# Attention on one Trainium2 core: V stationary, the work behind exp one tile later, and the output scaled by GpSimd

## The chip, the cores and the metric

The kernel runs on one NeuronCore of one Trainium2 chip. The metric is the device time of one execution in microseconds (us), the median of several runs. All durations of single instructions come from one profiled execution of the kernel before.

## What is computed

An attention over buckets, then two mixture-of-experts layers on its output. The change touches the attention alone, cut here to what matters:

```python
batch, n_heads, seq, head_dim = (2, 8, 768, 64)     # q, k, v float32; proj is 64 x 6
q_bits = (np.einsum('bhsd,dk->bhsk', q, proj) > 0)  # k_bits the same from k
mask = q_bucket[:, :, :, None] == k_bucket[:, :, None, :]
scores = np.where(mask, scale * np.matmul(q, k.transpose(0, 1, 3, 2)), -1000000000.0)
attn = np.exp(scores - np.max(scores, axis=-1, keepdims=True))
attn = attn / (np.sum(attn, axis=-1, keepdims=True) + 1e-09)
out = np.matmul(attn, v)
```

Behind it come a layer of 8 experts with two per token and one of 8 experts with one per token, over 1536 tokens of 512 values.

## The kernel before

There are H = 16 pairs of batch and head, treated one after another ("head" below). A head has 768 rows of q, taken as QT = 6 tiles of 128 rows; n counts tiles over all heads, j within a head. Head 0 and head 15 are written out, the 14 between run in a loop of two heads a round (over_heads). Each engine has its own program, and the order within it is the order written; engines meet by semaphores.

For a tile, TensorE computes 128 x 768 scores into one of two PSUM banks (scores, L1059 and L1060: two matmuls for each half of 384 columns, in fp32r, where each value is held as a high and a low part). The bits of the bucket are further rows of the same product, so that scores of other buckets come out very negative. VectorE takes the row maximum and makes the scale and bias from it (stats, L722, L725, L728). ScalarE computes exp with the row sum (expo, L561) into one of two buffers "probs" (in the tile work). TensorE transposes the six 128 x 128 blocks of it into one PSUM tile (turn, L1071); ScalarE copies the first half to SBUF (evac, L569), and VectorE the second half in even tiles (L735), ScalarE in odd ones. Then TensorE multiplies by V (weigh, L1083): for each of six blocks, the transposed P block of 128 x 128 is the stationary operand and V, 128 x 64 in plain fp32, moves; an fp32 product is two instructions. After six tiles VectorE scales the whole head's output by the inverse row sums into x_sb (head_out, L749; the inverses at L739 and L741).

Between these, the next head is prepared in six units, one per tile (prep_unit, PREP): the units for k and q (two halves each) are three transposes (L1039), a copy of the high part by ScalarE (L554) and a subtraction for the low part by VectorE (L702, L706); each of q and k is loaded twice, side by side, so that the transposed rows fill both halves of the partitions. The last two units compute the sign bits of the projections by four matmuls (L1044 to L1048), and VectorE turns them into rows of the operands (L710, L713). GpSimd copies the high part of q once more (q_copy, L453).

On TensorE the order of a tile is: scores(n), prep unit j of the next head, weigh(n - 2), turn(n - 1). On VectorE: stats, inverse sums, prep unit, head_out, evac. On ScalarE: copy of the prep unit, exp, evac. SP's queue issues the loads of q and k of the head after next (L328), the load of V (L331), and once in two heads the clears: 1 MB and 0.5 MB to xs (L352) and 1 MB to ys (L348), from a tile of zeros. After the last head, the routing of the first layer starts once x_sb is written; ScalarE and GpSimd then split the first expert's weights (L618, L463).

## Time and profile before

| | us |
|---|---|
| median of 3 runs | 1034.82 (1034.65 to 1037.06) |
| the profiled execution | 1035.75 |
| its span, first to last instruction | 1033.9 |
| PE busy in the span | 936.5 |
| VectorE busy | 587.9 |
| GpSimd busy | 410.1 |
| ScalarE busy | 340.3 |
| attention, first scores to the last write of x_sb | 16.95 to 347.63 |

The profiled execution is 1.85 us longer than its span. Busy time is the union of an engine's instructions. PE is TensorE's matmuls, PEld its weight loads, which overlap them; DVE is VectorE, ACT ScalarE, POOL GpSimd, SP the engine that issues most DMAs. A matmul's end in the trace is modelled, so the distance from one start to the next is the better measure of what it costs in a stream. L and a number is a line of the kernel before.

### The profile page before, as it was taken

The numbers are of one execution on the slowest core, as the hardware profiler recorded it, in microseconds if no ns is written. First come the engines' busy times: TensorE is split into PE (matmuls) and PEld (weight loads), VectorE is DVE, ScalarE is ACT, GpSimd is POOL, SyncE is SP. The second block draws the span as 40 slices with busy tenths as digits, with TensorE's granted clock in tenths as the row PEclk, the third lists the DMA queues.
The fourth block names the chain that finished last, engine by engine and source line by source line (L and its number), as shares of the span: only waits on it lengthen the run. The fifth ranks groups of instructions, "written<-read, shape, count | busy, mean of one in ns | idle before, by whom it ended". The sixth has DMA issues, their size and how long they took to land. (4 is left out here: it accounts for less than half of the span.)

```text
span 1033.9 us, 19204 instructions
## 1 busy us (share of the span) xinstructions
PE 936.5 (91%) x5502; PEld 793.0 (77%) x5503; DVE 587.9 (57%) x1136; ACT 340.3 (33%) x548; POOL 410.1 (40%) x251
## 2 busy tenths in 40 slices
PE   6999999999999938999999999999854999999980
PEld 4889988988898726888888888888643788888860
DVE  5777777777777474544445544454367454444432
ACT  2655555565555410422121111120212134342000
POOL 1000000000000547966152433331955889896004
PEclk9999999999999967999999999999976999999995
DMA  8351543435514525655252534332765677774107
GB/s 264 95 156 38 147 138 70 139 89 124 142 38 171 203 98 207 238 191 189 75 181 84 170 102 141 122 131 87 231 210 189 216 239 254 234 252 147 47 31 243
DMA packets 116173, 158.31 MB, mean 153 GB/s; under 512 B 57904, under 2 KB 59952, under 8 KB 116144
## 3 DMA queue, kind: packets, MB, share of 16 engines
q1 hardware_dynamic: 83280, 70.37, 22.3%
q10 hardware_dynamic: 26624, 67.12, 19.9%
q0 software_dynamic: 6240, 20.45, 6.1%
q8 instruction: 16, 0.26, 0.1%
q14 instruction: 13, 0.11, 0.0%
HBM read 104.43 MB, written 53.48 MB: 153 GB/s over the span
## 5 line engine op out<-in xcount | busy, mean ns | idle before, releaser
L463 POOL TENSOR_TENSOR wring<-stage,wring 128x1024 f32 (+1 forms) x128 | 302.3, 2395 | 197.1 <-ACT wring L618 197.0
L618 ACT ACTIVATE wring<-stage 128x1024 f32 (+1 forms) x128 | 135.4, 1061 | 429.7 <-POOL wring L463 213.8
L1203 PE MATMUL bank<-wring,xT_hl 128*128 x352 | 142.7, 405 | 5.2 <-DVE xT_hl L936 5.2
L1083 PE MATMUL bank<-raw,work 128*128 128x64 f32 x1152 | 143.6, 275 | 3.2 <-ACT work L569 3.2
L1083 PEld LDWEIGHTS bank<-raw,work 128*128 128x128 f32 x1152 | 135.9, 191 | 12.9 <-issue 10.9
L1220 PE MATMUL bank<-wring,hT_hl 128*128 x352 | 141.6, 402 | 3.2 <-DVE hT_hl L955 3.2
L453 POOL TENSOR_TENSOR wring<-wring,ones 64x384 fp32r<-64x384 f32 x32 | 26.2, 819 | 287.3 <-ACT wring L554 287.3
L1205 PE MATMUL bank<-wring,xT_hl 128*128 x352 | 138.8, 394 | 0.0
L1204 PE MATMUL bank<-wring,xT_hl 128*128 x352 | 137.9, 392 | 0.0
L1222 PE MATMUL bank<-wring,hT_hl 128*128 x352 | 137.8, 391 | 0.0
L1221 PE MATMUL bank<-wring,hT_hl 128*128 x352 | 137.1, 390 | 0.0
L962 DVE COPY work<-bank 128x512 f32<-128x512 f32 x44 | 30.5, 694 | 178.2 <-PE bank L1222 168.5
L561 ACT ACTIVATE work<-bank,stat 128x768 f32<-128x768 f32 x96 | 95.2, 991 | 101.8 <-DVE stat L728 101.8
L722 DVE TENSOR_REDUCE stat<-bank 128x1 f32<-128x768 f32 x96 | 91.8, 956 | 59.7 <-PE bank L1060 58.5
L943 DVE TENSOR_SCALAR work<-bank 128x512 f32<-128x512 f32 x88 | 60.9, 692 | 108.2 <-PE bank L1205 108.2
L1203 PEld LDWEIGHTS bank<-wring,xT_hl 128*128 128x128 f32 x352 | 66.8, 190 | 18.6 <-issue 6.2
L1071 PE MATMUL bank<-ident,work 128*128 128x128 f32 x576 | 79.9, 275 | 0.6 <-ACT work L569 0.6
L1220 PEld LDWEIGHTS bank<-wring,hT_hl 128*128 128x128 f32 x352 | 66.1, 188 | 16.1 <-issue 3.7
L1205 PEld LDWEIGHTS bank<-wring,xT_hl 128*128 128x128 f32 x352 | 66.6, 189 | 14.8
L1222 PEld LDWEIGHTS bank<-wring,hT_hl 128*128 128x128 f32 x352 | 66.1, 188 | 14.7
L1204 PEld LDWEIGHTS bank<-wring,xT_hl 128*128 128x128 f32 x352 | 67.0, 190 | 13.0
L1221 PEld LDWEIGHTS bank<-wring,hT_hl 128*128 128x128 f32 x352 | 66.3, 188 | 12.7
(171 smaller groups left out, 1290.6 us busy)
## 6 DMA issues: line engine op xcount, KB each, us to landing
stage<-in_moe_w_dram ACTq DMA_DIRECT2D x128, 512.0 KB, 4.0
ys<-work SPq DMA_DIRECT2D x44, 256.0 KB, 3.4
work<-xs SPq DMA_DIRECT2D x40, 256.0 KB, 3.5
xs<-stage SPq DMA_DIRECT2D x7, 1024.0 KB, 4.5
ys<-stage SPq DMA_DIRECT2D x7, 1024.0 KB, 8.2
raw<-in_k_dram SPq DMA_DIRECT2D x32, 192.0 KB, 3.6
raw<-in_q_dram SPq DMA_DIRECT2D x32, 192.0 KB, 3.8
xs<-stage SPq DMA_DIRECT2D x7, 512.0 KB, 5.2
```

Of the source, the lines that this page charges most:

```text
L463: nc.gpsimd.tensor_tensor(wring[:, bass.ds(at + DC * F, GW)], stage[:, j % STAGES, :], wring[:, bass.ds(at, GW)].bitcast(F32), ALU.subtrac ...
L561: nc.scalar.activation(probs[par].rearrange("p (b c) -> p b c", b=2), s_ps[par][:, :, 0:HALF], ACT.Exp, bias=stat[:, par, 2:3], scale=stat ...
L618: nc.scalar.activation(wring[:, bass.ds(parity * SLOT + high_at(j), GW)], stage[:, j % STAGES, :], ACT.Copy).then_inc(w_high, 1)
L722: vec.tensor_reduce(stat[:, par, 0:1], s_ps[par][:, :, 0:HALF], AX.XY, ALU.max).then_inc(s_max, 1)
L1071: ins = nc.tensor.transpose(pt_ps[:, half, i * P:(i + 1) * P], probs[par][:, c:c + P], ident[:])
L1083: ins = mm(o_ps[:, j * D:(j + 1) * D], probsT[j % 2][:, i * P:(i + 1) * P], vraw[:, hp, i], start=i == 0, stop=i == QT - 1)
L1203: mm(o, xT_hl[:, 0, c, :], wh, start=c == 0, stop=False)
L1204: mm(o, xT_hl[:, 0, c, :], wl, start=False, stop=False)
L1205: ins = mm(o, xT_hl[:, 1, c, :], wh, start=False, stop=c == DC - 1)
L1220: mm(y_ps[:], hT_hl[:, 0, c, :], wh, start=c == 0, stop=False)
L1221: mm(y_ps[:], hT_hl[:, 0, c, :], wl, start=False, stop=False)
L1222: ins = mm(y_ps[:], hT_hl[:, 1, c, :], wh, start=False, stop=c == FC - 1)
```

## The change

V is split by GpSimd into a high and a low part side by side (v_hl, 128 columns) and becomes the stationary operand; three tiles' transposed P, also split into high and low (pT_top by ScalarE, pT_rest by VectorE), moves, 384 columns at a time. The result is the transposed output of three tiles, its two halves of 64 partitions to be added. ScalarE copies it (o_copy), a product with the matrix "fold" transposes it back and adds the halves (turn_back), ScalarE copies that out of PSUM (o_evac), and GpSimd scales it into x_sb (head_out). turn, the evacuations and all behind them run for tile n - 2 where they ran for n - 1. q and k are loaded once, side by side, and transposed together in two units; the high and low parts are put in their places by seven DMAs from SBUF to SBUF per head (put_split, put_bits), for which the first scores of a head wait. The sign bits take three matmuls per half and one VectorE instruction. The maximum is taken negated, and its product with the scale is a tensor_tensor. The parts of the diff that matter are these, added lines alone, less indented; what they take the place of stands in the functions printed above (semaphore names and the constants of the start are left out):

```diff
+qk_raw = raw[:, 0:2].rearrange("p a t d -> p (a t d)").rearrange("p (t x) -> p t x", x=2 * D)
...
+qk_top = ring_part(11)
+qk_rest = ring_part(12)
+late = wring[:, SLOT:2 * SLOT]
+TRIO = 3 * P
+pT_top = [late[:, i * QT * TRIO:(i + 1) * QT * TRIO].rearrange("p (c n) -> p c n", n=TRIO) for i in (0, 1)]
+pT_rest = [late[:, i * QT * TRIO:(i + 1) * QT * TRIO].rearrange("p (c n) -> p c n", n=TRIO) for i in (2, 3)]
+v_hl = [late[:, (16 + i) * S:(17 + i) * S].rearrange("p (c x) -> p c x", x=2 * D) for i in range(2)]
...
+o_flat = [work[:, 2 * S + i * TRIO:2 * S + (i + 1) * TRIO] for i in range(2)]
+fold = work[:, 3 * S:3 * S + D]
+o_raw = [work[:, 3 * S + D + i * KH * D:3 * S + D + (i + 1) * KH * D].rearrange("p (t d) -> p t d", d=D)
+         for i in range(2)]
...
+o_ps = banks[3][:, 0, 0:TRIO]
+misc_ps = banks[3][:, 1, :]
...
+U = 4
+PUTS = 7
+S_O0 = 2
...
+        for at, t in ((0, q), (D, k)):
+            sp.dma_start(qk_raw[:, :, at:at + D], head_rows(t, h)).then_inc(qk_ld, 16)
+    def put(to, at, n, t, row):
+        sp.dma_start(to[at:at + n, :].bitcast(F32), t[row:row + n, :].bitcast(F32)).then_inc(qk_put, 16)
+    def put_split(h, par):
+        sp.wait_ge(prep_ev, h * U + 2)
+        put(q_hl[par], 0, D, qk_top, 0)
+        put(k_hh[par], 0, D, qk_top, D)
+        put(q_hl[par], D, D, qk_rest, 0)
+        put(k_hh[par], D, D, qk_top, D)
+        put(q_hb[par], 0, D, qk_top, 0)
+        put(k_lb[par], 0, D, qk_rest, D)
+    def put_bits(h, par):
+        sp.wait_ge(prep_ev, h * U + 4)
+        put(q_hb[par], D, 2 * BITS, k_lb[par], QB)
...
+    put_split(0, 0)
+    put_bits(0, 0)
+    def next_head(h, par):
+        put_split(h + 1, 1 - par)
+        load_qk(h + 2)
+        put_bits(h + 1, 1 - par)
+        sp.wait_ge(v_rdy, h * 2 + 2)
+        load_v(h + 2, par)
+            next_head(i * 2 + par, par)
+    put_split(H - 1, 1)
+    put_bits(H - 1, 1)
...
+    def split_v(h, par, part):
+        c = slice(part % 2 * KH, (part % 2 + 1) * KH)
+        vr = vraw[:, par, c]
+        if part < 2:
+            if part == 0:
+                pool.wait_ge(v_ld[par], (h // 2) * 16 + 16)
+                if not (isinstance(h, int) and h < 2):
+                    pool.wait_ge(s_pv, h * 2 - 2)
+            one = ones[:, 0:KH * D].rearrange("p (c d) -> p c d", d=D) if KH * D <= P else \
+                ones[:, 0:1].unsqueeze(1).broadcast_to([P, KH, D])
+            nc.gpsimd.tensor_tensor(v_hl[par][:, c, 0:D], vr, one, ALU.mult).then_inc(v_top, 1)
+        else:
+            pool.wait_ge(v_top, h * 2 + (part - 1))
+            nc.gpsimd.tensor_tensor(v_hl[par][:, c, D:2 * D], vr, v_hl[par][:, c, 0:D].bitcast(F32),
+                                    ALU.subtract).then_inc(v_rdy, 1)
+    def head_out(h, hp, half):
+        pool.wait_ge(o_out, h * 2 + (half + S_O0 + 1))
+        pool.wait_ge(s_rinv, h * 2 + 2)
+        xs = x_sb[:].rearrange("p b t h d -> p (b t) (h d)")
+        to = xs[:, bass.ds(h // HB * QT + half * KH, KH), bass.ds(h % HB * D, D)]
+        nc.gpsimd.tensor_tensor(to, o_raw[half],
+                                rinv[:, hp, half * KH:(half + 1) * KH].unsqueeze(2).broadcast_to([P, KH, D]),
+                                ALU.mult).then_inc(s_o, 1)
+    def head(h, hp):
+        for j in range(4):
+            split_v(h, hp, j)
+        if not first(h):
+            for half in range(2):
+                head_out(h - 1, 1 - hp, half)
+    over_heads(pool, head)
+    for half in range(2):
+        head_out(H - 1, 1, half)
...
+    def top_part(h, u):
+        act.wait_ge(prep_mm, h * U + (u + 1))
+        nc.scalar.activation(qk_top[:, cols(u)], prep_bank(h, u)[:, 0:HALF], ACT.Copy).then_inc(prep_top, 1)
...
+    def pT_high(n, hh, j):
+        for half in range(2):
+            act.wait_ge(pt_mm, n * 2 + (half + 1))
+            if half == 0 and not (isinstance(hh, int) and hh < 2):
+                act.wait_ge(s_pv, hh - 1)
+            at = j % KH * P
+            nc.scalar.activation(pT_top[j // KH][:, half * KH:(half + 1) * KH, at:at + P],
+                                 pt_ps[:, half, 0:HALF].rearrange("p (c n) -> p c n", n=P),
+                                 ACT.Copy).then_inc(pt_top, 1)
+    def o_copy(hh, par):
+        act.wait_ge(s_pv, hh + 1)
+        nc.scalar.activation(o_flat[par], o_ps, ACT.Copy).then_inc(o_cp, 1)
+    def o_evac(hh, half):
+        act.wait_ge(o_back, hh + 1)
+        act.wait_ge(s_o, hh + (S_O0 - 1))
+        nc.scalar.activation(o_raw[half], misc_ps[:, 0:KH * D].rearrange("p (t d) -> p t d", d=D),
+                             ACT.Copy).then_inc(o_out, 1)
+    for u in range(2):
+        top_part(0, u)
+            if j >= 2:
+                pT_high(n - 2, h * 2 + (j - 2) // KH, j - 2)
+            elif not first(h):
+                pT_high(n - 2, h * 2 - 1, QT - 2 + j)
+            if j in (1, 4) and not first(h):
+                o_copy(h * 2 - (2 if j == 1 else 1), 0 if j == 1 else 1)
+            if not last(h) and j < 2:
+                top_part(h + 1, j)
+            if not first(h) and j >= U:
+                o_evac(h * 2 - 2 + (j - U), j - U)
...
+    link(vec.tensor_tensor(fold, ident[:, 0:D], ident[:, D:P], ALU.add))
...
+        half = u % 2
+        if u < 2:
+            dve.wait_ge(prep_top, h * 2 + (u + 1))
+            ins = vec.tensor_tensor(qk_rest[:, c], bank[:, 0:HALF], qk_top[:, c].bitcast(F32), ALU.subtract)
+            b = slice(D, PW)
+            ins = vec.tensor_scalar(k_lb[par][b, c], bank[b, 0:HALF], bit_rule[b, 2:3], bit_rule[b, 3:4],
+                                    ALU.is_gt, ALU.mult)
...
+        vec.tensor_reduce(stat[:, par, 0:1], s_ps[par][:, :, 0:HALF], AX.XY, ALU.max,
+                          negate=True).then_inc(s_max, 1)
+        dve.wait_ge(s_max, n + 1)
+        vec.tensor_scalar(stat[:, par, 1:2], stat[:, par, 0:1], BIG / 2, SCALE, ALU.is_lt,
+                          ALU.mult).then_inc(s_scale, 1)
+        dve.wait_ge(s_scale, n + 1)
+        vec.tensor_tensor(stat[:, par, 2:3], stat[:, par, 0:1], stat[:, par, 1:2],
+                          ALU.mult).then_inc(s_stat, 1)
+    def pT_low(n, j):
+        dve.wait_ge(pt_top, n * 2 + 2)
+        at = j % KH * P
+        vec.tensor_tensor(pT_rest[j // KH][:, :, at:at + P].rearrange("p (b c) n -> p b c n", b=2),
+                          pt_ps[:, :, 0:HALF].rearrange("p b (c n) -> p b c n", n=P),
+                          pT_top[j // KH][:, :, at:at + P].bitcast(F32).rearrange("p (b c) n -> p b c n", b=2),
+                          ALU.subtract).then_inc(pt_rdy, 1)
...
+            if j >= 2:
+                pT_low(n - 2, j - 2)
+            elif not first(h):
+                pT_low(n - 2, QT - 2 + j)
+            if not last(h) and j < U:
+            if not first(h):
+                if j == U - 1:
+                    inverse_sums(h - 1, 1 - hp)
+    for j in (QT - 2, QT - 1):
+        pT_low((H - 1) * QT + j, j)
...
+        half = u % 2
+            if u:
+                pe.wait_ge(prep_ev, h * U + u)
+            elif not (isinstance(h, int) and h < 2):
+                pe.wait_ge(o_out, h * 2 - (4 - S_O0))
+        if u < 2:
+                pe.wait_ge(qk_ld, h * 32 + 32)
+                ins = nc.tensor.transpose(bank[:, i * P:(i + 1) * P], qk_raw[:, half * KH + i], ident[:])
+            to = bank[0:PW, 0:HALF]
+            mm(to, p_h, qk_top[:, c], start=True, stop=False)
+            mm(to, p_h, qk_rest[:, c], start=False, stop=False)
+            ins = mm(to, p_l, qk_top[:, c], start=False, stop=True)
+        if j == 0:
+            pe.wait_ge(qk_put, h * (16 * PUTS) + 16 * PUTS)
+            pe.wait_ge(prep_ev, h * U + U)
...
+        if not (isinstance(n, int) and n < 1):
+            pe.wait_ge(pt_rdy, n)
+    def weigh(hh, b, h, hp, part):
+        if part == 0:
+            pe.wait_ge(v_rdy, h * 2 + 2)
+            pe.wait_ge(pt_rdy, hh * KH + KH)
+            if not (isinstance(hh, int) and hh == 0):
+                pe.wait_ge(o_cp, hh)
+        for i in (2 * part, 2 * part + 1):
+            mm(o_ps, v_hl[hp][:, i], pT_top[b][:, i], start=i == 0, stop=False)
+            ins = mm(o_ps, v_hl[hp][:, i], pT_rest[b][:, i], start=False, stop=i == QT - 1)
+        if part == 2:
+            ins.then_inc(s_pv, 1)
+    def turn_back(hh, b, h):
+        pe.wait_ge(o_cp, hh + 1)
+        if b:
+            pe.wait_ge(o_out, h * 2 + (S_O0 + 1))
+        elif isinstance(h, int) and h >= H - 2:
+            pe.wait_ge(o_out, h * 2 + S_O0)
+        else:
+            pe.wait_ge(prep_ev, h * U + 3 * U)
+        for i in range(KH):
+            ins = mm(misc_ps[:, i * D:(i + 1) * D], o_flat[b][:, i * P:(i + 1) * P], fold, start=True, stop=True)
+        ins.then_inc(o_back, 1)
+    for u in range(2):
+    for u in range(2, U):
+        if u == 2:
+            pe.wait_ge(dve_c, 20)
+            if j >= 2:
+                turn(n - 2, j % 2)
+            elif not first(h):
+                turn(n - 2, j % 2)
+            if j == QT - 1:
+                weigh(h * 2, 0, h, hp, 0)
+            elif not first(h):
+                if j < 2:
+                    weigh(h * 2 - 2, 0, h - 1, 1 - hp, j + 1)
+                else:
+                    weigh(h * 2 - 1, 1, h - 1, 1 - hp, j - 2)
+            if not last(h) and j < U:
+            if not first(h) and j >= U:
+                turn_back(h * 2 - 2 + (j - U), j - U, h - 1)
+    turn(H * QT - 2, 0)
+    weigh(2 * H - 2, 0, H - 1, 1, 1)
+    turn(H * QT - 1, 1)
+    weigh(2 * H - 2, 0, H - 1, 1, 2)
+    turn_back(2 * H - 2, 0, H - 1)
+    for part in range(3):
+        weigh(2 * H - 1, 1, H - 1, 1, part)
+    turn_back(2 * H - 1, 1, H - 1)
```

## Rows read from the trace of the kernel before

**Rows 1.** The page, part 1: busy us (share of the span) x instructions.

```profile
PE 936.5 (91%) x5502; PEld 793.0 (77%) x5503; DVE 587.9 (57%) x1136; ACT 340.3 (33%) x548; POOL 410.1 (40%) x251
```

**Rows 2.** Stretches: length, busy PE, PEld, DVE, ACT, POOL, granted clock, DMA share, GB/s.

```profile
200.00:330.00 130.00, 128.69 (x965) 116.49 (x966) 98.14 (x204) 75.96 (x157) 9.83 (x12) 1.00 0.39 112
...
370.00:385.00 15.00, 1.30 (x25) 1.06 (x25) 12.55 (x47) 2.83 (x4) 4.12 (x3) 0.55 0.28 105
```

**Rows 3.** Timeline, VectorE at the first tile of heads 1 and 15: start, us, instruction.

```profile
38.52 0.96 DVE L722 TENSOR_REDUCE stat<-bank 128x1 f32<-128x768 f32 x1 [0.15 <-PE bank L1060]
...
39.81 0.17 DVE L739 TENSOR_SCALAR rinv<-rsum 128x6 f32<-128x6 f32 x1
...
327.36 0.16 DVE L739 TENSOR_SCALAR rinv<-rsum 128x6 f32<-128x6 f32 x1
```

**Rows 4.** Timeline, TensorE's weight loads over one tile.

```profile
201.82 0.19 PEld L1059 LDWEIGHTS bank<-wring 128*128 128x128 f32 x1
...
202.49 0.42 PEld L1039 LDWEIGHTS bank<-ident,raw 128*128 128x128 f32 x3
...
202.88 1.42 PEld L1083 LDWEIGHTS bank<-raw,work 128*128 128x128 f32 x12
...
204.17 0.69 PEld L1071 LDWEIGHTS bank<-ident,work 128*128 128x128 f32 x6
...
204.83 0.19 PEld L1059 LDWEIGHTS bank<-wring 128*128 128x128 f32 x1
```

**Rows 5.** Timeline, from the first load of a unit of bits to the next work.

```profile
214.86 0.17 PEld L1044 LDWEIGHTS bank<-wring 128*108 128x108 f32 x1
...
216.35 1.41 PEld L1083 LDWEIGHTS bank<-raw,work 128*128 128x128 f32 x12 [0.19 <-issue]
```

**Rows 6.** Groups of instructions from 45 to 325 us: busy us, mean ns | idle before.

```profile
L561 ACT ACTIVATE work<-bank,stat 128x768 f32<-128x768 f32 x82 | 81.3, 991 | 87.8 <-DVE stat L728 87.8
L722 DVE TENSOR_REDUCE stat<-bank 128x1 f32<-128x768 f32 x82 | 78.4, 956 | 50.5 <-PE bank L1060 49.5
...
L728 DVE SCALAR_TENSOR_TENSOR stat<-stat 128x1 f32<-128x1 f32 x82 | 23.7, 289 | 2.8
...
L713 DVE TENSOR_SCALAR wring<-bank,bit_rule 12x384 fp32r<-12x384 f32 x28 | 19.2, 687 | 0.4
...
L706 DVE TENSOR_TENSOR wring<-bank,wring 64x384 fp32r<-64x384 f32 x27 | 15.1, 561 | 0.8
```

**Rows 7.** Timeline: P's transposes and evacuations; GpSimd beside VectorE.

```profile
22.86 0.56 DVE L706 TENSOR_TENSOR wring<-bank,wring 64x384 fp32r<-64x384 f32 x1
22.90 0.82 POOL L453 TENSOR_TENSOR wring<-wring,ones 64x384 fp32r<-64x384 f32 x1 [9.73 <-ACT wring L554]
...
201.16 0.70 PEld L1071 LDWEIGHTS bank<-ident,work 128*128 128x128 f32 x6
...
201.80 0.49 ACT L569 ACTIVATE work<-bank 128x384 f32<-128x384 f32 x1 [0.51 <-PE bank L1071]
...
205.30 0.86 ACT L569 ACTIVATE work<-bank 128x384 f32<-128x384 f32 x2
...
206.75 0.82 POOL L453 TENSOR_TENSOR wring<-wring,ones 64x384 fp32r<-64x384 f32 x1 [13.33 <-ACT wring L554]
...
207.03 0.55 DVE L728 SCALAR_TENSOR_TENSOR stat<-stat 128x1 f32<-128x1 f32 x1
```

**Rows 8.** SP's issues in the timeline; DMA issues: KB each, median us to landing.

```profile
212.72 1.25 SPq L328 DMA_DIRECT2D raw<-in_k_dram  x2
...
233.27 2.12 SPq L328 DMA_DIRECT2D raw<-in_k_dram  x2
...
ys<-stage SPq DMA_DIRECT2D x7, 1024.0 KB, 8.2
raw<-in_k_dram SPq DMA_DIRECT2D x32, 192.0 KB, 3.6
```

**Rows 9.** Timeline: the first scores, the last maximum, the last write of x_sb.

```profile
16.95 0.69 PE L1059 MATMUL bank<-wring 128*128 128x384 f32 x1
...
340.50 0.96 DVE L722 TENSOR_REDUCE stat<-bank 128x1 f32<-128x768 f32 x1 [1.34 <-PE bank L1060]
...
347.07 0.56 DVE L749 TENSOR_TENSOR x_sb<-bank,rinv 128x384 f32<-128x384 f32 x1 [3.25 <-PE bank L1083]
```

More of the change, by code:

```diff
@@ L112, in lsh_attention_two_moes @@
         PW = QB + 2 * BITS
[L113 to L115 removed]
+        p_f = work[:, 0:PW]
+        p_h, p_l = (ring_part(8 + i)[:, 0:PW] for i in range(2))
         wg_sb = [sb("wg0", [P, DC, 2 * E]), sb("wg1", [P, DC, E])]
@@ L289, in last @@
             return isinstance(h, int) and h == H - 1
-        PREP = [("k", 0), ("q", 0), ("k", 1), ("q", 1), ("bits", 0), ("bits", 1)]
-        U = len(PREP)
-        assert QT == U
+        U = 4
+        PUTS = 7
+        S_O0 = 2
         def prep_bank(h, u):
-            return o_ps if first(h) and u % 2 else prep_ps
+            return banks[3][:, 0, :] if first(h) and u % 2 else misc_ps
         def cols(half):
@@ L581, in head @@
                     n = h * QT + j
-                    if not last(h):
-                        copy_unit(h + 1, 1 - hp, j)
+                    if j >= 2:
[6 more added lines that the diff above has]
+                        top_part(h + 1, j)
                     expo(n, j % 2, j, hp)
-                    if j or not first(h):
-                        evacs(n - 1, (j - 1) % QT)
+                    if not first(h) and j >= U:
+                        o_evac(h * 2 - 2 + (j - U), j - U)
             over_heads(act, head)
-            evacs(H * QT - 1, QT - 1)
+            for j in (QT - 2, QT - 1):
+                pT_high((H - 1) * QT + j, 2 * H - 1, j)
+            for half in range(2):
+                o_copy(2 * H - 2 + half, half)
+                o_evac(2 * H - 2 + half, half)
             def expert_at(m, e):
@@ L1065, in turn @@
                 pe.wait_ge(s_exp, n + 1)
+                if not (isinstance(n, int) and n < 1):
+                    pe.wait_ge(pt_rdy, n)
                 for half in range(2):
-                    if not (isinstance(n, int) and n < 1):
-                        pe.wait_ge(pt_b if half else pt_a, n)
                     for i in range(KH):
```

161 lines of the change are left out of this document (22 added, 139 removed).

## The prediction

> **What bounds it now.** I read the page first. PE is busy for 91% of the span and no other engine for more than 57% [rows 1], but that is a mean over stages, so the next view was the table by stretches. In the attention stage PE is busy for 128.7 of 130 us, VectorE for 98 and ScalarE for 76 [rows 2]: the stage is a stream of TensorE work and the others have room. The edits lie in this stage alone. One head takes (327.36 - 39.81) / 14 = 20.54 us [rows 3].
>
> What a tile is made of I took from the timeline, by start to start of the weight loads [rows 4]: scores 0.67, one prep unit of three transposes 0.39, the product with V (12 instructions of 64 columns, half of its time spent on loading P as weights) 1.29, the six transposes of P 0.66; together 3.01 us. A unit of sign bits takes 1.49 [rows 5]. Per head: 6 x (0.67 + 1.29 + 0.66) + 4 x 0.39 + 2 x 1.49 = 20.3 us, against 20.54 measured. So PE's stream is the bound, and 0.25 us are waits.
>
> **PE after the change.** V (high and low part side by side, 128 columns) is stationary, and the product moves 3 x 128 columns of P: 12 matmuls of the scores' size for three tiles, four per tile, so 0.67 us [rows 4] in place of 1.29. Scores and transposes of P stay. The q and k transposes shrink from four units to two (0.39 each). The bit units have three matmuls for four: 1.49 x 3/4 = 1.1 each. The turn back is three fp32 products, six instructions, twice a head: 6 x 1.29 / 12 = 0.65 each. Per head: 6 x (0.67 + 0.66 + 0.67) + 0.78 + 2.2 + 1.3 = 16.3 us. PE alone would save 4.2 us per head, 67 us over 16.
>
> **ScalarE.** Exp stays (0.99 [rows 6]). P's evacuation is 0.87 per tile for two halves [rows 7], before one and a half. Per head there are two top parts and two output copies at about 0.45 and two PSUM copies of 192 columns at about 0.3. That is 6 x 1.86 + 2.4 = 13.6 us: it is not the bound, but it sits in the loop below.
>
> **VectorE** gains the big term. The maximum and its two small instructions take 39.81 - 38.52 = 1.29 [rows 3]. The new low part of P reads 768 columns from PSUM and one SBUF operand. No row shows that; the nearest is the maximum over 768 columns, 0.956 [rows 6]. Below, it can hardly be under that; above, twice the 384-column bit instruction gives 1.37 [rows 6]. I take 0.96. Per head: 6 x (1.29 + 0.96) + 2 subtractions over 384 columns at 0.56 [rows 6] + 2 bit instructions at 0.69 + inverse sums 0.34 = 16.3 us. So VectorE and PE come out level, and how they hand over decides.
>
> **The loop.** P's transposes have one PSUM tile, and it is now free only when the low part is made. Transposes, high part (ScalarE), low part (VectorE), next transposes: 0.64 from the first weight load to the start of the evacuation, 0.87 evacuation, some 0.15 hand-over, 0.96 low part [rows 6, 7] = 2.62 us. Walking the head's tiles in the order in which each engine is programmed: tiles 0 and 1 are set by VectorE, 1.29 + 0.96 + 0.56 = 2.81 each; tile 2 also, 1.29 + 0.96 + 0.69 = 2.94; tile 3 too with the inverse sums, 3.28; tiles 4 and 5 by PE with the turn back, 3 x 0.67 + 0.65 = 2.65, level with the loop. Sum 17.14 us. Scores have two banks, so they do not wait on ScalarE: exp of tile n ends some 3.5 us after tile n begins, and scores n+2 are wanted after 5.
>
> **GpSimd against VectorE.** GpSimd goes from two instructions per head of 64x384 (0.82 us) to six of 128x192: the four V splits and the two scalings. In the trace the GpSimd instruction at 206.75 holds VectorE's two-operand 128x1 instruction until 207.58: 0.55 instead of 0.16 [rows 7], and the mean of that instruction is 0.289 [rows 6], so 82 x 0.13 / 27 = 0.39 us are lost per GpSimd instruction. The changed kernel keeps a two-operand SBUF instruction in that place, so six could cost 2.3 us per head; none can cost less than zero. At the head's start, where the four splits lie, VectorE has 0.3 us to spare before P's evacuation ends. I take 0.5. The forecast is 17.6 us per head.
> The Trainium skill (SBUF — State Buffer, Who interferes with whom) has GpSimd and a VectorE instruction with two SBUF inputs share a read interface by an exclusive lock, and an instruction with one SBUF input outside the two-port modes not contending. By it the new low part (one operand in PSUM) goes free and the small product alone pays; the trace agrees, since the subtraction at 22.86, with one operand in PSUM, takes its usual 0.56 beside GpSimd's instruction at 22.90 [rows 7].
>
> **SP and the DMAs.** Loads of q and k fall from four to two per head; seven SBUF to SBUF transfers are added: six of 64 rows x 3 KB (192 KB) and one of 12 rows. The first scores of a head now wait for all seven. Six are issued after the second prep evacuation, about 6 us into the head, at 0.62 each, up to 1.06 when the queue is full of clears [rows 8], so until 9.7 to 12.4; two loads behind them until 11 to 14.5; the last transfer, wanted from 12.0 on, then goes out at 12.6 to 15 and lands 3.6 later by the loads' median [rows 8], at 16.2 to 18.7. The first scores are wanted at 16.5. So it is near: hidden in heads without clears, up to 2 us late in every second head at the worst. I price it at nothing and put the 2 us x 7 = 14 us into the range. V's load waits for the split of a V that arrived a head before, and the clears behind it on SP's queue drain in some 9 us [rows 8], before the next head's transfers are issued.
>
> **Ends.** Start: the first scores begin at 16.95 [rows 9]. The new chain has two loads fewer ahead (1.3 us), two prep units fewer, and then six issues and a landing: I work out 19. The first head has no P work in its first two tiles, and ends about as before or up to 3 us sooner; I take -1, between +4 and -4. The last head: five tiles at 2.65 for 14.4 before, -1. Tail: from the last maximum to the last write of x the trace has 347.63 - 340.50 = 7.1 us [rows 9]. The new tail is serial: two loops of 2.62, copy 0.5, turn back 0.65, twelve matmuls 2.0, copy 0.5, turn back 0.65, PSUM copy 0.3, GpSimd scaling 0.35 to 0.82, hand-overs 0.15 each: 12.6 us, +5.5. ScalarE and GpSimd begin the first expert's weights 1.6 us later against the routing, under a wait of over 10 us that GpSimd has there anyway.
>
> **Sum.** 14 middle heads x (17.6 - 20.54) = -41.2; -1 -1 +5.5: -37.7 us. The profiled execution took 1035.75; 998.0. The median of the runs is 0.9 lower: 997.
>
> **Rivals.** First, VectorE is the bound and dearer than I have it: the low part nearer to 1.37, or GpSimd holding it 2.3 us per head. For it: no row prices either. Against: the 384-column subtraction with an operand in SBUF costs no more than half a maximum over 768 and a start-up [rows 6]. A low part of 1.1 in six tiles and 2 us of blocking make 17.6 + 0.85 + 1.5 = 20.0 at most, typically 18.9: 1015, between 1005 and 1030.
>
> Second, slower: the transfers between partitions set the head's period. The place is the wait before a head's first scores. If the last of the seven lands by 16.5 us it costs nothing; each us beyond is a us per head, and from 2.5 us on (about 3 with the ends) the gain is gone. If six transfers of 64 rows drain as slowly as the clear of 1 MB does, 8.2 us to landing [rows 8], the last one lands at 21: +4.5 x 15 = 67 us, 1065.
> The Trainium skill (SBUF — State Buffer, Door 1: The DMA port swizzle) speaks against the change here: 64 partitions reach half of the ports, 196 GB/s, so an estimate by that page is 1 us a transfer, 6 us for the six. By it the last would land near 17, half a us late: 7 us over all. No row here has a transfer of 64 partitions.
>
> Third, the clock. PE now has holes of about 7% per head. The granted clock was 1.00 in the stage at 99% busy and 0.55 in the routing, where PE was busy for 1.3 of 15 us [rows 2]. Should holes of 0.4 us let it fall to 1.2 GHz for a quarter of the stage, the PE stream there doubles: +16 x 14 / 4 = 56 us, about 1053. Against: the holes are short, and half the clock fills them.
>
> Fourth, it does nothing: what attention gains, the next stage waits for (clears, weights). The clears move in bursts with gaps between, and GpSimd waits in routing, so 2%.
>
> **Chances.** Forecast (990 to 1005) 0.55; better still (no blocking, a quicker start, 980 to 990) 0.08; first rival 0.23; second 0.06 slower, and 0.02 in a mild form near no change; third 0.04; fourth 0.02. Range 984 to 1022, which leaves out the slow rivals and the far end of the first. A measurement of this kernel can tell 0.3%, 3.1 us. Faster 0.86, same 0.04, slower 0.10.
>
> **What would show it.** Right: heads 17.6 us apart by the inverse sums; PE busy 92% in the stage at clock 1.00; the product's matmuls at 0.17 spacing; the low part 0.96; the idle time of P's transposes ended by the low part; the 128x1 product sometimes at 0.4 or more. Wrong: the first scores of a head released by a DMA, a low part of over 1.1, a clock under 1.00 in the stage, a tail over 13 us.

## The result and the profile after

The changed kernel takes 997.15 us (median of 4 runs, 995.35 to 998.70) against 1034.74 (4 runs, 1034.05 to 1037.06): 0.963 of the time before, 95% interval 0.961 to 0.9655. The profiled execution took 997.38 us, its span 995.6. Forecast were 997 for the median and 998.0 for the profiled execution. One execution each of changed_again, product_twice and three_edits below came in a slow state (1519, 1640 and 2920 us); the ratios are of the others.

The page's busy times, to be held against [rows 1]:

```profile
PE 873.6 (88%) x4798; PEld 739.7 (74%) x4799; DVE 595.6 (60%) x1104; ACT 365.9 (37%) x628; POOL 433.0 (43%) x315
```

The attention's loop, with the columns of [rows 2]:

```profile
45.00:285.00 240.00, 226.92 (x1503) 205.92 (x1502) 221.93 (x418) 189.49 (x417) 41.54 (x82) 1.00 0.69 186
```

In the stage PE was busy 99% of the time and VectorE 75% [rows 2]. Now PE has 94.5%, VectorE 92.5%, ScalarE 79%, at a granted clock of 1.00: two engines are level, with a third near them.

The costly groups of that stretch, with the columns of [rows 6]. L806 is the low part of P, L630 its high part, L1136 P's transposes, L1147 and L1148 the product with V, L785 the bits, L507 GpSimd's scaling, L495 and L498 its splits of V:

```profile
L620 ACT ACTIVATE work<-bank,stat 128x768 f32<-128x768 f32 x83 | 82.3, 992 | 18.2 <-DVE stat L800 17.8
L794 DVE TENSOR_REDUCE stat<-bank 128x1 f32<-128x768 f32 x84 | 80.0, 952 | 8.7 <-PE bank L1125 7.9
L806 DVE TENSOR_TENSOR wring<-bank,wring 128x768 fp32r<-128x768 f32 x83 | 79.3, 956 | 1.7 <-ACT wring L630 1.1
L630 ACT ACTIVATE wring<-bank 128x384 fp32r<-128x384 f32 x168 | 73.5, 492 | 22.9 <-PE bank L1136 22.9
L1136 PE MATMUL bank<-ident,work 128*128 128x128 f32 x501 | 70.4, 276 | 13.1 <-DVE wring L806 12.0
...
L800 DVE TENSOR_TENSOR stat<-stat 128x1 f32<-128x1 f32 x84 | 19.2, 229 | 2.9
```

The low part, which no row of before priced, takes 0.956 us; 0.96 was taken. What PE now waits for is the low part, as forecast.

The timeline of one head, a part of tile 0 and then tiles 2 to 5: PE's weight loads and some of the work of VectorE, GpSimd and SP (start, us, instruction):

```profile
198.57 0.37 DVE L800 TENSOR_TENSOR stat<-stat 128x1 f32<-128x1 f32 x1
198.87 0.94 DVE L806 TENSOR_TENSOR wring<-bank,wring 128x768 fp32r<-128x768 f32 x1
...
198.89 1.14 POOL L498 TENSOR_TENSOR wring<-raw,wring 128x192 fp32r<-128x192 f32 x2
...
203.03 3.76 SPq L348 DMA_DIRECT2D wring<-wring  x6
203.17 0.19 PEld L1147 LDWEIGHTS bank<-wring 128*128 128x128 f32 x1
...
203.81 0.17 PEld L1110 LDWEIGHTS bank<-wring 128*108 128x108 f32 x1
...
204.33 0.19 PEld L1124 LDWEIGHTS bank<-wring 128*128 128x128 f32 x1
...
205.91 0.96 DVE L794 TENSOR_REDUCE stat<-bank 128x1 f32<-128x768 f32 x1
...
207.10 0.16 DVE L800 TENSOR_TENSOR stat<-stat 128x1 f32<-128x1 f32 x1
207.21 0.96 DVE L806 TENSOR_TENSOR wring<-bank,wring 128x768 fp32r<-128x768 f32 x1
...
208.20 0.69 DVE L785 TENSOR_SCALAR wring<-bank,bit_rule 44x384 fp32r<-44x384 f32 x1
...
208.91 0.85 SPq L348 DMA_DIRECT2D wring<-wring  x1
...
208.91 0.17 DVE L813 TENSOR_SCALAR rinv<-rsum 128x6 f32<-128x6 f32 x1
...
209.34 0.96 DVE L794 TENSOR_REDUCE stat<-bank 128x1 f32<-128x768 f32 x1
...
212.51 0.51 POOL L507 TENSOR_TENSOR x_sb<-work,rinv 128x192 f32 x1 [12.47 <-ACT work L641]
...
212.68 0.36 DVE L800 TENSOR_TENSOR stat<-stat 128x1 f32<-128x1 f32 x1
...
213.67 0.19 PEld L1124 LDWEIGHTS bank<-wring 128*128 128x128 f32 x1
...
214.70 0.96 DVE L794 TENSOR_REDUCE stat<-bank 128x1 f32<-128x768 f32 x1 [0.55 <-PE bank L1125]
```

Tile 3 goes from maximum to maximum in 209.34 - 205.91 = 3.43 us without a gap on VectorE: 1.30 until the low part, then the low part, the bits and the inverse sums. Measured like this, and averaged over heads 3 to 14, the six tiles take 2.77, 2.72, 2.99, 3.43, 2.16 and 3.20 us; the fourth (tile 3) is the longest. The product with V starts at 203.17 and the next work at 203.81, 0.64 for 0.67 forecast. The last transfer is issued at 208.91, and the next head's first scores load at 213.67, behind the turn back, not behind a DMA.

Where the 38.2 us of the attention's end went, by the starts of the maxima (heads 0, 1 and 15) and the last one (296.91) and the last write of x_sb:

| | before | after | difference | forecast |
|---|---|---|---|---|
| to the first maximum of head 1 | 38.52 | 40.11 | +1.6 | -1 |
| 14 middle heads | 287.58 | 243.66 | -43.9 | -41.2 |
| one head | 20.54 | 17.27 (heads 3 to 14) | -3.27 | -2.94 |
| last head | 14.40 | 13.14 | -1.3 | -1 |
| tail | 7.1 | 12.5 | +5.4 | +5.5 |
| sum | 347.63 | 309.40 | -38.2 | -37.7 |

The span fell by 38.3: nothing of it was given back behind the attention. The 14 middle heads include head 1, which took 19.07 us, 1.8 more than the others.

The start and the tail in the timeline:

```profile
19.65 0.69 PE L1124 MATMUL bank<-wring 128*128 128x384 f32 x1 [7.99 <-DMA wring<-wring]
...
25.24 6.34 SPq L348 DMA_DIRECT2D wring<-wring  x6
...
33.28 0.84 SPq L348 DMA_DIRECT2D wring<-wring  x1
...
38.43 0.68 PE L1124 MATMUL bank<-wring 128*128 128x384 f32 x1 [3.36 <-DMA wring<-wring]
...
43.07 0.33 PEld L1125 LDWEIGHTS bank<-wring 76*128 76x128 f32 x1
43.39 0.33 PEld L1124 LDWEIGHTS bank<-wring 128*128 128x128 f32 x1
...
299.23 0.64 PEld L1136 LDWEIGHTS bank<-ident,work 128*128 128x128 f32 x6 [0.53 <-issue]
...
301.80 0.64 PEld L1136 LDWEIGHTS bank<-ident,work 128*128 128x128 f32 x6 [1.31 <-issue]
...
304.62 0.19 PEld L1147 LDWEIGHTS bank<-wring 128*128 128x128 f32 x1
...
307.02 0.49 ACT L636 ACTIVATE work<-bank 128x384 f32<-128x384 f32 x1 [1.81 <-PE bank L1148]
...
308.48 0.33 ACT L641 ACTIVATE work<-bank 128x192 f32<-128x192 f32 x1 [0.97 <-PE bank L1162]
308.89 0.51 POOL L507 TENSOR_TENSOR x_sb<-work,rinv 128x192 f32<-128x192 f32 x1 [3.10 <-ACT work L641]
```

Head 0 begins with a wait for its transfers (19.65, forecast 19). Of the 15 heads behind it, head 1 is the only one released by a DMA (38.43): the six issues at 25.24 take 6.34 us where they take 3.76 at 203.03, and from the start of the last issue (33.28) to the scores 5.15 us pass. After that hole PE runs at the lower of its two levels, 1.2 GHz:

```profile
38.40:44.00 5.60, 5.57 (x20) 5.39 (x21) 2.40 (x5) 1.68 (x4) 0.00 (x0) 0.50 0.01 4
```

Its loads are 0.32 us apart there (43.07, 43.39), for 0.18 at 2.4 GHz. From 45 us on the granted clock is 1.00. The tail is a serial chain, each step waiting for the one before.

### The profile page after: what moved, and what is told of

Same layout as the page of the kernel before. It is cut to its first block and busy times, and to the rows that moved or that the text cites. A ratio compares the mean times of both kernels' runs of the same rounds, so it can differ in the third digit from the quotient of the medians.

```text
span 995.6 us, 18018 instructions
## 1 busy us (share of the span) xinstructions
PE 873.6 (88%) x4798; PEld 739.7 (74%) x4799; DVE 595.6 (60%) x1104; ACT 365.9 (37%) x628; POOL 433.0 (43%) x315
## 5 line engine op out<-in xcount | busy, mean ns | idle before, releaser
L507 POOL TENSOR_TENSOR x_sb<-work,rinv 128x192 f32 (+1 forms) x32 | 16.3, 508 | 254.0 <-ACT work L641 254.0
L620 ACT ACTIVATE work<-bank,stat 128x768 f32<-128x768 f32 x96 | 95.2, 992 | 20.1 <-DVE stat L800 19.6
L1136 PE MATMUL bank<-ident,work 128*128 128x128 f32 x576 | 81.5, 278 | 19.0 <-DVE wring L806 17.1
L630 ACT ACTIVATE wring<-bank 128x384 fp32r<-128x384 f32 x192 | 84.1, 491 | 33.2 <-PE bank L1136 33.1
L806 DVE TENSOR_TENSOR wring<-bank,wring 128x768 fp32r<-128x768 f32 x96 | 91.7, 956 | 7.0 <-ACT wring L630 6.3
L1136 PEld LDWEIGHTS bank<-ident,work 128*128 128x128 f32 x576 | 63.5, 142 | 41.4 <-issue 38.4
L1124 PE MATMUL bank<-wring 128*128 128x384 f32 x192 | 72.1, 375 | 11.4 <-DMA wring<-wring 11.4
L1293 PEld LDWEIGHTS bank<-wring,xT_hl 128*128 128x128 f32 x352 | 66.9, 190 | 18.6 <-issue 6.1
L1310 PEld LDWEIGHTS bank<-wring,hT_hl 128*128 128x128 f32 x352 | 66.2, 188 | 16.1 <-issue 3.7
L1295 PEld LDWEIGHTS bank<-wring,xT_hl 128*128 128x128 f32 x352 | 66.7, 189 | 14.3
L1312 PEld LDWEIGHTS bank<-wring,hT_hl 128*128 128x128 f32 x352 | 66.1, 188 | 14.3
```

The lines of the kernel that those rows point to most:

```text
L620: nc.scalar.activation(probs[par].rearrange("p (b c) -> p b c", b=2), s_ps[par][:, :, 0:HALF], ACT.Exp, bias=stat[:, par, 2:3], scale=stat ...
L806: vec.tensor_tensor(pT_rest[j // KH][:, :, at:at + P].rearrange("p (b c) n -> p b c n", b=2), pt_ps[:, :, 0:HALF].rearrange("p b (c n) -> ...
L1136: ins = nc.tensor.transpose(pt_ps[:, half, i * P:(i + 1) * P], probs[par][:, c:c + P], ident[:])
L1293: mm(o, xT_hl[:, 0, c, :], wh, start=c == 0, stop=False)
L1295: ins = mm(o, xT_hl[:, 1, c, :], wh, start=False, stop=c == DC - 1)
L1310: mm(y_ps[:], hT_hl[:, 0, c, :], wh, start=c == 0, stop=False)
```

## The experiments

They ran on other chips, where the kernel before took 1059 to 1061 us. The changed kernel, run again there in the last group, gives the scale:

**changed_again**, the changed kernel as it is.

> The changed kernel itself, without an edit, on this chip beside the others: ratio 0.961 to 0.966, heads 17.26 us, head 1's first scores 3.4 us after the end of the work before them.

Measured: 1024.75 us, ratio 0.9649 (0.9629 to 0.9669) to the kernel before, and 17.27 us a head (heads 3 to 14); the hole before head 1 was 2.93 us, for 3.36. The ratio, within its interval, and the heads are those of the first chip; the extra time lies behind the attention (its last maximum starts at 295.4, against 296.91). So below ratios and head lengths are compared, 0.9649 and 17.27 being the changed kernel's. A ratio of 0.001 is 1.06 us there, and 1.03 in the times of the forecasts, which are on the first chip's scale. The intervals are 0.002 to 0.003 to each side: an edit worth under 4 us can't be told by the total. The head lengths tell more; they are means over heads 3 to 14 of one profiled execution, and the two executions of the changed kernel agree in them to 0.01 us.

### Which engine sets the head

**product_twice** gives PE about its old load of the product again and nothing to the others; each matmul of the product runs twice, with half the fold.

```diff
-mm(o_ps, v_hl[hp][:, i], pT_top[b][:, i], start=i == 0, stop=False)
-ins = mm(o_ps, v_hl[hp][:, i], pT_rest[b][:, i], start=False, stop=i == QT - 1)
+for again in range(2):
+    mm(o_ps, v_hl[hp][:, i], pT_top[b][:, i], start=i + again == 0, stop=False)
+    ins = mm(o_ps, v_hl[hp][:, i], pT_rest[b][:, i], start=False, stop=i + again == QT)
...
+link(vec.tensor_scalar(fold, fold, 0.5, None, ALU.mult))
```

> Edit: every matmul of the product with V is issued twice and the fold matrix is halved, so PE has four more matmuls per tile, 0.70 us, about what the old form of the product took more. Theory A (the shorter PE stream is where the gain comes from; PE has only some 1 us per head to spare): PE's stream per head becomes 15.9 + 4.1 = 20.0 to 20.4, heads 20.2 us apart, time 1040, so the gain over the kernel before is gone. Rival G (the gain comes from moving the work behind exp one tile later, and PE has room): heads under 18.5 us, time under 1015.

Measured: 1062.49 us, ratio 1.0012 (0.9995 to 1.0029); heads 19.77. Its stretch, same columns:

```profile
45.00:320.00 275.00, 275.00 (x1836) 270.97 (x1835) 219.79 (x419) 189.70 (x419) 42.65 (x84) 1.00 0.60 162
```

PE is busy in all of it, and the gain in time is gone, as theory A has it; rival G is excluded. The 24 further matmuls of a head at the 0.174 spacing of 203.81 to 204.33 are 4.2 us, and the head grows by 2.5. So PE's own stream in the changed kernel is 19.77 - 4.2 = 15.6 us, and the head of 17.27 holds 1.7 us in which PE waits (the busy share, in which the ends are modelled, shows 0.95).

**low_half** takes load off VectorE: the low part is made of half the columns.

```diff
-vec.tensor_tensor(pT_rest[j // KH][:, :, at:at + P].rearrange("p (b c) n -> p b c n", b=2),
-                  pt_ps[:, :, 0:HALF].rearrange("p b (c n) -> p b c n", n=P),
-                  pT_top[j // KH][:, :, at:at + P].bitcast(F32).rearrange("p (b c) n -> p b c n", b=2),
+vec.tensor_tensor(pT_rest[j // KH][:, 0:KH, at:at + P],
+                  pt_ps[:, 0, 0:HALF].rearrange("p (c n) -> p c n", n=P),
+                  pT_top[j // KH][:, 0:KH, at:at + P].bitcast(F32),
                   ALU.subtract).then_inc(pt_rdy, 1)
...
-ins = mm(o_ps, v_hl[hp][:, i], pT_rest[b][:, i], start=False, stop=i == QT - 1)
+ins = mm(o_ps, v_hl[hp][:, i], pT_rest[b][:, i % KH], start=False, stop=i == QT - 1)
```

> Edit: the low part of P is made for the first three of the six blocks only; the other three use it in their place (the low-part term of blocks 3 to 5 is left out of the result). PE has the same matmuls, VectorE's instruction shrinks from 768 to 384 columns, 0.4 us less per tile. Theory A (VectorE sets tiles 0 to 3): these tiles lose 0.25 to 0.4 us each until PE sets them, tiles 4 and 5 nothing; a head 16.0 to 16.3 us, time 980 to 984. Rival H (PE's stream or ScalarE's is the bound already): a head 17.0 or more, time over 993.

Measured: 995.34 us, ratio 0.940 (0.9381 to 0.942); heads 15.75. The low part's group and the stretch:

```profile
L806 DVE TENSOR_TENSOR wring<-bank,wring 128x384 fp32r<-128x384 f32 x84 | 46.6, 555 | 1.7 <-ACT wring L630 1.7
```

```profile
45.00:265.00 220.00, 218.99 (x1501) 208.52 (x1500) 188.92 (x419) 185.03 (x418) 41.40 (x82) 1.00 0.76 203
```

VectorE has 6 x 0.40 = 2.4 us less; the head falls by 1.5, until PE is busy 99.5% of the time. It ends a little under the 16.0 to 16.3 expected, and at PE's stream as product_twice gives it. Two runs from opposite sides agree: PE alone 15.6 to 15.75. The rest of the head is VectorE's. This run alone can't tell VectorE's own stream from the loop through the one PSUM tile, since the low part stands in both; the next one can, since the inverse sums stand in VectorE's stream alone.

**inverse_j4** moves the inverse sums, 209.34 - 208.91 = 0.43 us of VectorE's stream, from tile 3 to tile 4.

```diff
-if j == U - 1:
+if j == U:
     inverse_sums(h - 1, 1 - hp)
```

> Edit: VectorE's inverse sums of the head before stand in tile 4 instead of tile 3. Theory A (VectorE's own stream sets tiles 0 to 3, PE with the turn back sets tiles 4 and 5): tile 3 loses 0.43 us and tiles 4 and 5 hide it, so a head goes from 17.26 to 16.85 us and the time to 991 (6 us less). Rival D (VectorE is the bound of the whole head): the work is only moved, a head stays at 17.2 to 17.3 and the time within 1 us of 997. Rival E (the loop through the one PSUM tile sets every tile): also no change.

Measured: 1017.49 us, ratio 0.9601 (0.9575 to 0.9626); heads 16.91 (-0.36). Tile 3 falls from 3.43 to 3.00 us. Tile 4 grows from 2.16 to 2.47, but tile 5, in which VectorE waited for scores, shrinks by the same 0.31, from 3.20 to 2.89: the two together stay at 5.36, as PE sets them.

```profile
206.36 0.16 DVE L813 TENSOR_SCALAR rinv<-rsum 128x6 f32<-128x6 f32 x1
...
206.66 0.95 DVE L794 TENSOR_REDUCE stat<-bank 128x1 f32<-128x768 f32 x1
```

The same work costs its full length in a tile that VectorE sets and nothing in tiles that PE sets. (Tile 0 grew by 0.07 us: GpSimd's scaling no longer meets VectorE's small product in tile 5, and its splits hold the one in tile 0 for 0.40 where it was 0.34.) The total agrees, 0.9601 for 0.9649, with intervals that lie just apart.

### GpSimd beside VectorE

**one_operand** makes the 128x1 product a form that GpSimd may not hold.

```diff
-vec.tensor_tensor(stat[:, par, 2:3], stat[:, par, 0:1], stat[:, par, 1:2], ALU.mult)
+vec.tensor_scalar(stat[:, par, 2:3], stat[:, par, 0:1], stat[:, par, 1:2], None, ALU.mult)
```

> Edit: the product of maximum and scale becomes a tensor_scalar with the scale as per-partition scalar, so it has one tensor operand in SBUF. Theory A (GpSimd holds the two-operand form, mean 0.229 against 0.160, but where there is slack): the mean falls to about 0.155 and the time by 0 to 2 us. Rival F (GpSimd's holding costs the 0.5 us per head of the forecast): the time falls by 6 to 7 us, to 990.

Measured: 1021.71 us, ratio 0.9633 (0.9612 to 0.9654); heads 17.20 (-0.07). The product's group and, from the timeline, one of them with the low part behind it:

```profile
L800 DVE TENSOR_SCALAR stat<-stat 128x1 f32<-128x1 f32 x84 | 18.0, 214 | 3.0
```

```profile
205.34 0.21 DVE L800 TENSOR_SCALAR stat<-stat 128x1 f32<-128x1 f32 x1
205.47 0.95 DVE L806 TENSOR_TENSOR wring<-bank,wring 128x768 fp32r<-128x768 f32 x1
```

All 84 now take 212 to 216 ns: no blocking is left. But the form is dearer than an undisturbed tensor_tensor, whose median was 160 ns (mean 229, longest 469), and the mean did not fall to the 0.155 expected. In VectorE's stream it costs less than its length: the low part starts 0.13 behind it (205.34, 205.47), for 0.11 in the changed kernel (207.10, 207.21).

Where the blocking stood the changed kernel's trace shows. Of its 84 instructions 56 take 159 to 163 ns and 28 take 286 to 469, two in a head: one in tile 5 beside the first scaling (212.68) and one in tile 0 beside the splits of V (198.57). All of it is 6 x (0.229 - 0.160) = 0.41 us of VectorE's time per head. In tile 5 it fills time in which VectorE would wait anyway (0.55 us for scores at 214.70): without it the tile takes 3.19 for 3.20. In tile 0 it counts: 2.69 for 2.77. The other four tiles change by 0.02 or less. So some 0.1 us of the 0.41 reaches the head, and rival F, 0.5 us a head, is excluded.

### The delay by one tile

**one_tile_sooner** undoes it for the transposes and evacuations of P; the product with V stays where it is.

```diff
-if j >= 2: turn(n - 2, j % 2)
-elif not first(h): turn(n - 2, j % 2)
+if j >= 1 or not first(h): turn(n - 1, (j + 1) % 2)
...
-if j >= 2: pT_low(n - 2, j - 2)
+if j >= 1: pT_low(n - 1, j - 1)
...
-if j >= 2: pT_high(n - 2, h * 2 + (j - 2) // KH, j - 2)
+if j >= 1: pT_high(n - 1, h * 2 + (j - 1) // KH, j - 1)
...
```

> Edit: the transposes of P and all evacuations run for tile n - 1 again instead of n - 2; V stays stationary. Theory A (one tile later only takes the wait for exp out of the chain; with n - 1 the chain exp 1.0, transposes 0.64, evacuation 0.87 on ScalarE makes 2.55 per tile and ScalarE's other work of 2.4 us per head adds to it in part): heads 17.6 to 18.6 us, tail one loop of 2.6 us shorter, time 999 to 1013. Rival G (the shift is where the gain comes from): heads at 20 us or more, time over 1033. Rival I (the shift does nothing in the middle and costs a loop in the tail): heads 17.3, time 994.

Measured: 1053.11 us, ratio 0.9954 (0.9934 to 0.9974); heads 20.20. The waits from 45 to 285 us (waiting group <- releaser: us in total, times, longest):

```profile
PE bank L1136 <- ACT work L620: 46.5, 48, 1.6
ACT wring L630 <- PE bank L1148: 39.0, 23, 1.7
```

Two things are mixed here. P's transposes wait for their own exp, and twice a head ScalarE's evacuation waits for the end of the product (L1148), whose operand buffer it overwrites. The head is as long as rival G has it, but the second wait comes from the edit, not from the order of the kernel before, so this run doesn't decide. Another run moves the product and the output copy as well:

**all_one_tile_sooner** adds to it:

```diff
-if j == QT - 1: weigh(h * 2, 0, h, hp, 0)
+if j >= QT - 2: weigh(h * 2, 0, h, hp, j - (QT - 2))
...
-if j < 2: weigh(h * 2 - 2, 0, h - 1, 1 - hp, j + 1)
-else: weigh(h * 2 - 1, 1, h - 1, 1 - hp, j - 2)
+if j < 1: weigh(h * 2 - 2, 0, h - 1, 1 - hp, 2)
+else: weigh(h * 2 - 1, 1, h - 1, 1 - hp, j - 1)
...
-if j in (1, 4) and not first(h):
+if j in (0, 3) and not first(h):
...
```

> Edit: transposes, evacuations, product with V and output copy all run one tile sooner than in the changed kernel (n - 1), so that no evacuation stands behind the last part of a product in its own tile, as it did in one_tile_sooner. Theory A2 (of the 2.9 us per head of that run, some 2.1 came from those two waits, and the chain exp, transposes, evacuation of 2.5 us per tile costs the rest): heads 17.4 to 18.2 us, tail 2.6 us shorter, time 0.961 to 0.975 of the kernel before. Rival G2 (the one tile of delay itself is worth 2 us or more per head): heads 19.3 or more, ratio 0.985 or more.

Measured: 1042.18 us, ratio 0.9816 (0.9795 to 0.9837); heads 18.92. Its waits, same stretch:

```profile
ACT wring L630 <- PE bank L1136: 48.5, 76, 0.8
PE bank L1136 <- ACT work L620: 33.1, 51, 0.9
```

The wait for the product is gone and the head is 1.3 us shorter, but still 1.65 over the changed kernel: between the 18.2 of theory A2 and the 19.3 of rival G2, so neither forecast of the size was met. With the transposes directly behind the exp of the tile before, PE waits for ScalarE and ScalarE, before its next exp, for PE. In the changed kernel the wait of L1136 for L620 does not occur in the list. So of the gain of 3.27 us per head, 1.65 goes if the delay alone is undone and 2.5 if PE's load alone is put back; the two overlap, and with one of them missing 1.6 or 0.8 us of the gain are left.

### The transfers between partitions

**puts_in_halves** moves the same bytes by twelve transfers of 32 rows, not six of 64.

```diff
-sp.dma_start(to[at:at + n, :].bitcast(F32), t[row:row + n, :].bitcast(F32)).then_inc(qk_put, 16)
+for part in range(0, n, D // 2):
+    m = min(D // 2, n)
+    sp.dma_start(to[at + part:at + part + m, :].bitcast(F32),
+                 t[row + part:row + part + m, :].bitcast(F32)).then_inc(qk_put, 16)
...
-PUTS = 7
+PUTS = 13
```

> Edit: each of the six transfers of 64 rows is issued as two of 32 rows, same bytes, six issues more (about 3.7 us on SP's queue). Theory A (the last of the seven transfers lands 1 to 2 us before a head's first scores want it): heads wait 2 to 3 us more each, time 1025 to 1040. Rival J (there is more than 4 us to spare): no change, 996 to 998. Rival K (the transfers already set the head's period): every us of issue is paid, +3.7 x 14 = 52 us, 1049 or more.

Measured: 1050.11 us, ratio 0.9908 (0.9881 to 0.9936); heads of 18.7 to 20.3. SP's queue and the first scores of one head (lines count three further here):

```profile
189.08 7.63 SPq L350 DMA_DIRECT2D wring<-wring  x12
...
197.66 0.61 SPq L342 DMA_DIRECT2D raw<-in_k_dram  x1
198.38 0.85 SPq L350 DMA_DIRECT2D wring<-wring  x1
...
201.33 0.44 PE L1127 MATMUL bank<-wring 128*128 128x384 f32 x1 [1.40 <-DMA wring<-wring]
```

This is the slow rival's mechanism, brought about on purpose. The twelve issues take 7.63 us for 3.76, and the scores are released by the last transfer, 201.33 - 198.38 = 2.95 us after its issue began (2.8 to 3.4 in heads 2 to 14). In the changed kernel 213.67 - 208.91 = 4.76 us pass there: 1.4 to 2.0 us to spare, so rivals J and K are excluded. The issue count costs here, with the same bytes: 0.63 us each on SP's queue.

Theory A's 1025 is just reached: 0.9908 is 1025 on the first chip. Not all of the loss is the wait, though. Heads 4, 5 and 8 to 13 take 18.7 to 19.2 us, 1.5 to 1.9 over the changed kernel. Heads 2, 3, 6 and 7 take 19.95 to 20.3, and in each of these the granted clock is 0.50 for some 3.4 us, from 1 to 1.5 us behind a hole of 1.4 to 1.6 us; for head 6:

```profile
143.60:146.90 3.30, 3.30 (x14) 3.20 (x13) 2.24 (x5) 1.80 (x4) 0.53 (x1) 0.50 1.04 395
```

Each fall costs a further 1.0 to 1.4 us. The other nine of heads 2 to 14 begin with holes of 1.3 to 1.8 us and no fall; the runs don't show what decides.

**clears_last** takes the 4.5 MB of clears issued at the start away from it and issues them after head 14.

```diff
-for m in range(2):
-    clear(m, NT[m] - rest[m], rest[m])
-clear_y(0, NT[0] - rest[0], rest[0])
-clear_y(1, NTMIN[1], NT[1] - NTMIN[1])
...
 put_bits(H - 1, 1)
+for m in range(2):
+    clear(m, NT[m] - rest[m], rest[m])
+clear_y(0, NT[0] - rest[0], rest[0])
+clear_y(1, NTMIN[1], NT[1] - NTMIN[1])
```

> Edit: the first four clears (4.5 MB) are issued after the last head's transfers instead of before head 0's. Theory A (head 1's first scores wait for transfers that stand behind these clears on the same queue): the 3.4 us hole before head 1 goes, PE is not slowed to half speed at 38 to 44 us, and head 1 begins at about 36 where it began at 40; all in all 4 to 6 us faster than the changed kernel, 991 to 993. Rival B (the seven transfers are slow by themselves, clears or none): the hole stays within 0.5 us and the time within 1 us of 997. Rival C (the gain is given back because 4.5 MB now drain when the routing wants its data): head 1 sooner, total within 1 us of 997.

Measured: 1020.00 us, ratio 0.9609 (0.9582 to 0.9636). The six issues take their usual time again:

```profile
24.96 3.77 SPq L348 DMA_DIRECT2D wring<-wring  x6
...
35.50 0.35 PE L1125 MATMUL bank<-wring 128*128 128x384 f32 x1
```

Head 1's first scores (35.50; PE's lines count one further here) follow the work before them without a wait, and the granted clock is 1.00 from 38 to 45 us. Head 1 has its first maximum at 36.45 (39.22 in changed_again) and lasts 17.57 (18.47); the last maximum starts at 291.91 against 295.39, 3.5 us sooner, a little under the 4 to 6 expected. The middle heads are unchanged. So start and head 1 carry the cost of transfers queued behind clears, and of the half clock after the hole; rival B is excluded. Rival C is not: from the last maximum to the end the profiled executions take 726.9 us, for 724.0 in changed_again, but this part differs by as much between runs that edit nothing there (724.1 in inverse_j4, 726.0 in one_operand). Whether the whole gain reaches the total, the two ratios can't tell either, since their intervals overlap.

### Together

**three_edits** has clears_last, inverse_j4 and one_operand.

> The edits of clears_last, inverse_j4 and one_operand together. If their gains stand in different places they add up: theory A expects 984 to 988 us. If the middle is bound by the loop through the PSUM tile once the inverse sums are moved, or if the transfers come to set the period, less: 989 to 993.

Measured: 1006.95 us, ratio 0.9491 (0.9464 to 0.9518); heads 16.77; last maximum at 284.41. It beats both kernels: 5% below the kernel before and 1.6% below the changed one (0.9491 / 0.9649), with intervals that lie apart. Theory A's 984 to 988 are 0.951 to 0.955 of the kernel before; it comes out a little better. The head is 0.50 us shorter, where the two edits to it had given 0.36 and 0.07 alone.

**four_edits** adds all_one_tile_sooner to these.

> all_one_tile_sooner with the three edits of three_edits. If the sooner schedule costs a head less than 0.19 us it beats three_edits by its shorter tail of 2.6 us: ratio under 0.9466. Theory A2 expects heads 16.9 to 17.8 us against 16.77 and a ratio of 0.948 to 0.962.

Measured: 1037.34 us, ratio 0.9779 (0.9764 to 0.9794), outside the forecast; heads 18.56. The delay is worth 1.8 us a head here too.

## Why the prediction was right

**The bound moves from PE to PE and VectorE together.** Right. VectorE's sum was 16.3 and its busy time is 221.93 / 240 x 17.27 = 16.0. PE's was 16.3 and product_twice gives 15.6; its busy share is 94.5% for 92. The bit unit is more than all of that error: priced at three quarters of the old one, 1.1, it takes 204.33 - 203.81 = 0.52, twice a head. That changed nothing, since PE is not what these tiles wait for.

**The walk by tiles.** 17.14 was worked out, 17.27 came. From one start of P's transposes to the next (199.93, 202.56, 205.28, 208.28, 211.71, 214.32, 217.17) the tiles take 2.63, 2.72, 3.00, 3.43, 2.61 and 2.85, for 2.81, 2.81, 2.94, 3.28, 2.65 and 2.65. Errors of up to 0.2 of both signs cancel. inverse_j4 and low_half confirm which engine sets which tile.

**GpSimd's blocking.** This is the mis-sized term of the middle: 0.5 us a head was added for it, and about 0.1 reaches the head (one_operand). As VectorE time it was 0.41. The prediction knew that only a part would count, but put the slack at 0.3 us at the head's start, where the splits lie; it lies in tile 5, where the scaling is, and tile 0 has none. Without the term the forecast would have been the walk's 17.14 for 17.27.
The Trainium skill (SBUF — State Buffer, Who interferes with whom) lets a VectorE instruction with two SBUF inputs contend with a GpSimd instruction that reads SBUF, and one with a single SBUF input, outside the two-port modes, not. The trace agrees: L800 takes 0.36 beside GpSimd at 212.51, and the low part, with one input in PSUM, takes 0.94 at 198.87 beside GpSimd's splits at 198.89, for a mean of 0.956.

**The start.** Wrong in sign: -1 forecast, +1.6 measured. The step that failed is the first head's: it was judged by its work on the engines ("ends about as before or up to 3 us sooner"), while the row that slows an issue to 1.06 behind clears was used only for the middle heads, where it never struck. Of the 3.36 us of the hole 6.34 - 3.76 = 2.6 stand in the issues; behind them the last landing took 5.15 us for some 3 in the middle. With the clears taken away the hole and the slow issues are gone (clears_last). The forecast's own sign of being wrong, scores of a head released by a DMA, so came true once.

**The transfers.** Priced at nothing, and right for the middle: in heads 2 to 15 the scores are released by something else, with 1.4 to 2.0 us to spare. The slow rival (1065) needed the last landing 4.5 us late. What puts_in_halves shows as their price is the issue, 0.63 us each on SP's queue, and some 3 us from the last of them to the scores.
By the rate that the Trainium skill (SBUF — State Buffer, Door 1: The DMA port swizzle) gives for 64 partitions, 196 GB/s, the estimate was 1 us a transfer and half a us late in every head. The trace disagrees with the estimate, since no head from 2 on waits; no row shows the rate of a single transfer, so that figure is neither borne out nor refuted.

**The ends and the clock.** The last head (-1.3 for -1) and the tail (+5.4 for +5.5) came as priced. For the tail there is luck in it: the steps that the prediction lists add up to 10.2 to 10.7 us, under 12 with a hand-over of 0.15 behind each, not 12.6. The list leaves out the 2.32 us from the last maximum to the first of the two loops (296.91 to 299.23), and it counts a copy and a turn back that in the trace lie beside the second loop (301.80 to 304.62). The granted clock of the stage stayed at 1.00, with PE's holes at 0.5 us or less, so its rival fell. It was at half after the 3.36 us hole of head 1, and in puts_in_halves, with holes of about 1.5 us, it fell in four heads of 13: a part of that rival's price.

**The other rivals.** The low part took 0.956, not 1.1 to 1.37, which removes the first. That it does nothing is excluded by the span, 38.3 shorter for 38.2 in the attention.

That the total was within 0.2 us is partly luck: against the forecast +2.6 us at the start and -2.7 in the middle heads cancel, and in the middle the 1.5 us by which head 1 exceeds 17.6 hides a part of what the other 13 heads are shorter.

## What to carry to other kernels

When work leaves the engine that bounds a stage, add up the next engine's instructions tile by tile, in program order: the gain ends at that sum, and every small instruction then belongs in a tile that the other engine sets. Undoing or doubling one load at a time (PE's, VectorE's, the delay) shows what each is worth, and that the parts of a gain overlap. Transfers made of many small issues are paid on the queue that issues them: look at what stands ahead of them there, at the start above all.
